# Routed two-expert layer: per-chunk adds on GpSimd, and the last tile's transposes moved between two matmul halves

## The reference, cut to what matters

```python
def _moe2_ref(x, w_gate, w_noise, noise, w1, w2):      # N = 2304 tokens, D = 512, E = 8, F = 1024
    ...
    for e in range(E):
        for k in range(2):
            mask = top2[:, k] == e
            h = np.maximum(x[mask] @ w1[e], 0.0)
            out[mask] += top2_w[mask, k, None] * (h @ w2[e])
```

## Time and profile before

| | us |
|---|---|
| three runs | 1079.15, 1078.52, 1079.46 |
| their median | 1079.15 |
| the profiled execution's own time | 1079.31 |
| its span, first to last instruction | 1077.5 |
| PE busy | 1064.3 (99%) |
| DVE, ACT, POOL busy | 584.1, 332.9, 386.0 |
| granted clock of PE, mean | 0.999 of full speed |

### The profile page before, as it was taken

The page is one execution under the profiler, slowest core; times in us unless marked ns, Lnnn a source line. Parts: engine busy times, 40 slices in busy tenths (PEclk is TensorE's granted clock), DMA queues, the critical chain, the costliest instruction groups (busy, mean ns, idle before and its releaser), DMA issues.

```text
span 1077.5 us, 20101 instructions
## 1 busy us (share of the span) xinstructions
PE 1064.3 (99%) x6053; PEld 932.2 (87%) x6054; DVE 584.1 (54%) x1212; ACT 332.9 (31%) x735; POOL 386.0 (36%) x358
## 2 busy tenths in 40 slices
PE   8989999999999999999999999999999999999997
PEld 7878999999999999999988888888888888888886
DVE  6777334364363463453457775555565555556553
ACT  7997223242342432432352111020303020110222
POOL 4557991030030030120185425070706142240486
PEclk9999999999999999999999999999999999999999
DMA  8876535411311311211084535172616344332576
GB/s 228 272 239 207 172 92 184 130 60 28 119 59 30 117 59 30 97 59 30 25 252 158 154 89 165 39 209 44 195 49 162 81 123 124 87 94 49 158 238 238
DMA packets 199635, 133.18 MB, mean 124 GB/s; under 512 B 128752, under 2 KB 161408, under 8 KB 199584
## 3 DMA queue, kind: packets, MB, share of 16 engines
q1 hardware_dynamic: 177728, 75.14, 25.7%
q10 hardware_dynamic: 16032, 38.47, 11.2%
q0 software_dynamic: 5824, 18.95, 5.1%
HBM read 85.87 MB, written 42.73 MB: 119 GB/s over the span
## 4 chain that ended last, share of the span: by engine, by line
PE 97%; ACT 1%; DVE 1%; issue 0%; DMA 0%; SPq 0%; ACTq 0%
PE bank L863 28%; PE bank L1023 22%; PE bank L1044 22%; PE bank L895 14%; PE bank L1057 3%; PE bank L807 2%; PE bank L834 2%; PE bank L817 1%; PE bank L801 1%; ACT p_sb L1197 1%; PE bank L940 1%; DMA k_sb<-in_kT 0%; PE bank L919 0%; PE bank L876 0%; DVE token_rows_b L1859 0%
## 5 line engine op out<-in xcount | busy, mean ns | idle before, releaser
L863 PE MATMUL bank<-x_parts,mlp_weights 128*128 128x384 f32 x1704 | 309.3, 336 | 0.0
L863 PEld LDWEIGHTS bank<-x_parts,mlp_weights 128*128 128x128 f32 x1704 | 298.2, 188 | 5.3
L1023 PE MATMUL bank<-expert_parts,xT_high 128*128 (+1 forms) x688 | 216.5, 396 | 0.0
L1044 PE MATMUL bank<-expert_parts,hT_high 128*128 (+1 forms) x688 | 212.1, 389 | 1.4 <-DVE hT_low L1785 1.4
L722 POOL TENSOR_TENSOR expert_parts<-raw_expert_a,expert_parts 128x512 fp32r<-128x512 f32 x64 | 81.5, 1306 | 234.6 <-ACT expert_parts L1362 232.3
L895 PE MATMUL bank<-mlp_weights,hidden_parts 128*128 128x512 f32 x648 | 162.0, 394 | 0.0
L1044 PEld LDWEIGHTS bank<-expert_parts,hT_high 128*128 128x128 f32 x688 | 129.0, 188 | 28.6 <-issue 2.0
L1023 PEld LDWEIGHTS bank<-expert_parts,xT_high 128*128 128x128 f32 x688 | 125.7, 188 | 24.4 <-issue 0.4
L895 PEld LDWEIGHTS bank<-mlp_weights,hidden_parts 128*128 128x128 f32 x648 | 120.1, 188 | 23.2 <-issue 1.0
L1023 PE MATMUL bank<-expert_parts,xT_low 128*128 (+1 forms) x344 | 134.3, 390 | 0.0
L1044 PE MATMUL bank<-expert_parts,hT_low 128*128 (+1 forms) x344 | 134.1, 390 | 0.0
(11 more groups left out here) (214 smaller groups left out, 1232.1 us busy)
## 6 DMA issues: line engine op xcount, KB each, us to landing
raw_expert_a<-in_w ACTq DMA_DIRECT2D x32, 512.0 KB
raw_expert_b<-in_w ACTq DMA_DIRECT2D x32, 512.0 KB, 4.2
x_row<-routed_rows SPq DMA_DIRECT2D x172, 64.0 KB
expert_rows<-y_row SPq DMA_DIRECT2D x43, 256.0 KB
expert_rows<-zeros SPq DMA_DIRECT2D x4, 2304.0 KB, 11.3
v_sb<-in_v SPq DMA_DIRECT2D x32, 256.0 KB, 3.5
q_sb<-in_qT SPq DMA_DIRECT2D x15, 288.0 KB, 3.7
k_sb<-in_kT SPq DMA_DIRECT2D x15, 288.0 KB, 4.0
```

The source lines that it names most:

```text
L863: last = nc.tensor.matmul(bank[:, 0:CHUNK], w_sb[:, i, wp, at:at + P], xp[:, par, part, k, :], start=n == 0, stop=n == 3 * KB - 1)
L1023: last = nc.tensor.matmul(ps[half][:, 0:512], (xTh, xTl)[xp][:, buf, k, :], ew_sb[:, bass.ds(slot, 1), wp, k * F2 + half * 512:k * F2 + ha ...
L1044: last = nc.tensor.matmul(y_bank(t)[:, 0:D], (hTh, hTl)[hp][:, f, :], ew_sb[:, bass.ds(slot, 1), 2 + wp, f * D:(f + 1) * D].rearrange("p a ...
```

## The change

The diff in full but for the semaphores' declarations (`second_in` now has six, `last_second_in` and `last_mixed` are gone, `second_tile_half_done` is called `half_done`):

```diff
@@ POOL
             for c in range(CHUNKS):
-                if c == CHUNKS - 1:
-                    add(c - 1)
                 stored = entry(pool, T_NEED + c, 16 * 64)
                 pool.wait_ge(places, 1)
                 pool.wait_ge(y_row_out, stored)
-                if c < CHUNKS - 1:
-                    gather_chunk(c, 1, second_in[c])
-                else:
-                    for t in range(CHUNK_TILES):
-                        gather(chunk_rows(c, 1)[:, t, :], slots_u[:, CHUNK_TILES * c + t, 1:2], last_second_in[t])
+                gather_chunk(c, 1, second_in[c])
                 if c + 2 < CHUNKS:
                     gather_chunk(c + 2, 0, first_in[c + 2])
-                if 1 <= c < CHUNKS - 1:
-                    add(c - 1)
+                if c < CHUNKS - 2:
+                    add(c)
+            add(CHUNKS - 2)
+            add(CHUNKS - 1)
@@ PE
-            return ps[4] if isinstance(t, int) and t == 2 else ps[5]
+            return ps[4] if isinstance(t, int) and t in (2, ETILES - 1) else ps[5]
...
-                if not (isinstance(t, int) and t in (0, 2)):
+                if not (isinstance(t, int) and t in (0, 2, ETILES - 1)):
                     pe.wait_ge(y_row_done, ONE + t)
...
-            tile(ETILES - 2, (ETILES - 2) % 2)
-            now = tile(ETILES - 1, (ETILES - 1) % 2)
-            pe_hT(pe, ETILES - 1)
-            pe_down2(pe, ETILES - 1, *now)
+            before = tile(ETILES - 2, (ETILES - 2) % 2)
+            t = ETILES - 1
+            now = entries(t)
+            pe_hT(pe, t - 1)
+            pe_up2(pe, t, t % 2, *now)
+            pe_down2(pe, t - 1, *before, (0,))
+            pe_hT(pe, t)
+            pe_down2(pe, t - 1, *before, (1,))
+            pe_down2(pe, t, *now)
@@ ACT
+            def store_chunk(c):
+                act.wait_ge(rows_added, CHUNK_TILES * (c + 1))
+                act.dma_start(out_rows(c), chunk_rows(c, 1)).then_inc(rows_out, 16)
+
             for c in range(CHUNKS):
-                if c < CHUNKS - 1:
-                    scale(c, 1, second_in, second_scaled)
+                scale(c, 1, second_in, second_scaled)
                 if c + 2 < CHUNKS:
                     scale(c + 2, 0, first_in, first_scaled)
-                if c >= 1:
-                    act.wait_ge(rows_added, CHUNK_TILES * c)
-                    act.dma_start(out_rows(c - 1), chunk_rows(c - 1, 1)).then_inc(rows_out, 16)
+                if c < CHUNKS - 2:
+                    store_chunk(c)
+            store_chunk(CHUNKS - 2)
             c = CHUNKS - 1
             for t in range(CHUNK_TILES):
-                act.wait_ge(last_mixed, t + 1)
+                act.wait_ge(rows_added, CHUNK_TILES * c + t + 1)
                 act.dma_start(out_rows(c)[:, t, :], chunk_rows(c, 1)[:, t, :]).then_inc(rows_out, 16)
@@ DVE
-                if isinstance(t, int) and t == 2 and b == 0:
-                    dve.wait_ge(second_tile_half_done, 1)
+                if isinstance(t, int) and t in (2, ETILES - 1) and b == 0:
+                    dve.wait_ge(half_done, 1 if t == 2 else 2)
...
             dve_hT(dve, t - 1)
             dve_relu(dve, t)
+            dve_hT(dve, t, (0,))
             dve_y(dve, t - 1)
-            dve_hT(dve, t)
+            dve_hT(dve, t, (1,))
             dve_y(dve, t)
-            dve.wait_ge(first_scaled, CHUNK_TILES * CHUNKS)
-            for t in range(CHUNK_TILES):
-                dve.wait_ge(last_second_in[t], 16)
-                n, row = CHUNK_TILES * c + t, chunk_rows(c, 1)[:, t, :]
-                nc.vector.scalar_tensor_tensor(out=row, in0=row, scalar=kept[:, 1, n:n + 1],
-                                               in1=chunk_rows(c, 0)[:, t, :], op0=ALU.mult, op1=ALU.add
-                                               ).then_inc(last_mixed, 1)
```

More of the change, by code:

```diff
@@ L346, in attention_moe_kernel @@
         tile_done = sem("tile_done")
-        second_tile_half_done = sem("second_tile_half_done")
+        half_done = sem("half_done")
         y_row_done = sem("y_row_done")
@@ L354, in attention_moe_kernel @@
         first_in = [sem(f"first_in_{i}") for i in range(CHUNKS)]
-        second_in = [sem(f"second_in_{i}") for i in range(CHUNKS - 1)]
-        last_second_in = [sem(f"last_second_in_{t}") for t in range(CHUNK_TILES)]
-        last_mixed = sem("last_mixed")
+        second_in = [sem(f"second_in_{i}") for i in range(CHUNKS)]
         first_scaled = sem("first_scaled")
@@ L1047, in pe_down2 @@
                         n += 1
-            last.then_inc(tile_done if halves[-1] == 1 else second_tile_half_done, 1)
+            last.then_inc(tile_done if halves[-1] == 1 else half_done, 1)
         def pe_hT(pe, t):
```

## The result

The changed kernel's median is 1080.7 us (22 runs, 1079.62 to 1083.26) against 1079.64 for the kernel before (22 runs, 1078.52 to 1080.87). The ratio is 1.0014, with a 95% interval of 1.0008 to 1.0019: 1.1 us slower at the first, small but clear of noise. The forecast was 1.4 us faster, with nearly all its chance on "the same" or better, and the time lies above its range. The profiled execution took 1082.46 us, with a span of 1080.6.

A forecast was written before the change was run, and what follows sets the result against it. It took PE (99% busy), then the tail through DVE's adds and the last store, with POOL's gathers close beside, as the bound. The earlier PE and POOL ends let stores finish 1.4 us sooner: 1079.15 - 1.4 = 1077.7 us, range 1076.2 to 1079.7.

The forecast's parts named there:

- the first part: Opening on what bounds the kernel: PE 99% busy, then DVE's adds, the last store at 1075.0, SP's wait until 1077.0.
- part 3: Stores at the end: output data finishes near 1075.15 instead of 1076.55, 1.4 us gained.
- Part 1: Tile 42's transposes move between the halves of tile 41's product; PE's last matmul ends at 1070.5, 1.7 us earlier.
- a shorter PE tail alone would run into their landing: At the end, PE finishing sooner would still meet the landing of chunk 5's second rows, gathered at 1067.57 to 1071.0.
- Part 2: POOL's adds follow their own chunk; chunk 5's adds end at 1073.36, last store issued at 1073.39, 1.6 us earlier.
- Nothing moves: POOL's adds of chunks 0 and 1: chunk 1's is ready at 1029.73, when POOL was adding at 1029.79 anyway.
- No slack: Chunk 5's add at 1069.60: all three rows wait for one semaphore, so a later landing counts in full.
- A rule against the change: Skill's port-sharing rule: DVE's copy of tile 42 would block POOL's chunk 5 adds, adding 0.7 us, giving 1078.4; left out.
- Rival A: Short landings of second rows: chunks 3 and 4 land in 3.6 to 3.8 us, 0.9 faster, 1076.8; chance 0.20.
- Rival B: Long landings before POOL's adds of chunks 3 and 4: 2.45 us more, 1080.2; chance 0.16.
- Rival C: Only the last landing or the output's backlog: chunk 4's store goes late, gain only 0.3 us, 1078.9; chance 0.08.
- D: Second bank's split comes late behind `dve_y(41)`, PE idles again; POOL still decides, 1077.7 stays; no chance given.

The follow-up runs named there:

- first session: The changed kernel's first 22 runs against the kernel before: 1080.7 us, ratio 1.0014.
- in the second: The changed kernel, nothing altered, run again for a second trace: 1083.17 us (5 runs), ratio 1.0038 to the kernel before.
- single executions: The changed kernel, nothing altered, three more times with one run and a trace each: 1083.12, 1083.56 and 1085.61 us.
- transposes alone: The kernel before with only the diff's PE part and its DVE part, the three scale-and-adds still on DVE: 1080.15 us, ratio 1.0005.

## Why the prediction was wrong

**The step that failed** is in the first part: "SP leaves its wait at 1077.0, 0.5 before the span's end". From it I took the last store as what sets the end, and in part 3 gained 1.4 us by making that store earlier. Two things ended there at once. SP's wait was one; POOL's drain, over at 1077.2, was the other, and the change moves exactly POOL's last instruction, from 1071.0 to 1073.4 by my own working. With the drain in the sum it reads 1073.4 + 6.1 + 0.2 = 1079.7 against 1077.5: 2.2 us slower instead of 1.4 faster. Measured were 1.1 us slower in the first session, 3.2 in the second and 2.5 to 5.0 in the single executions. So the drain turns the sign; the size then hangs on when the last add ends. Some 0.5 us of the distance to the forecast is none of the change's: the forecast started from a median of 1079.15 in three runs, and 22 runs gave 1079.64.

Point by point:
- Part 1 was right: PE's end and tile 42's copy came 1.6 us earlier (1.7 said). It was cover that made it worthless, and "a shorter PE tail alone would run into their landing" is what the kernel with the transposes alone shows.
- Part 2's chain came out within 0.6 us in the first trace and the second (969.2 and 969.9 against 969.6), and 2.2 to 4.8 us short in the three single executions. In the first trace that is in part luck: it started 1.7 us earlier, because tile 37 was copied earlier, and lost 0.9 of that on chunk 1. "Nothing moves" for chunk 1 was wrong in four of the five traces: its landing of 3.79 was one trace's. Of the other two that were taken over, chunk 3's (4.39) is in the middle of what the five traces gave and chunk 4's (4.20) at the low end. "No slack" was right as a warning, but the largest overruns were on chunks 2 and 3: 7.0 and 6.2 us in the slowest trace.
- Part 3: in the first trace the stores were through at 1076.7, or 1075.1 by the clock of before: the working gives about 1075.6 (data to 1075.15, and the wait left 0.4 behind them). The stores' gain was 1.9 us where 1.4 were said, and they were no longer the last.
- "A rule against the change", which I left out of the sum, would have put 0.7 us on the adds. Nothing of that shows: six adds took 7.49 us with tile 42's copy, out of PSUM, in the middle of them, which is twice 3.75.
- Rival A didn't happen: chunks 3 and 4 took 4.0 us and more in each of the five traces. Rival B did in the three single executions, on top of the drain: 2.2, 2.2 and 4.8 us, where its price was 2.45. The one trace of the first session doesn't show it. I gave it 0.16 and priced it on chunks 3 and 4 alone, while chunks 1 and 2 overran as well. Rival C couldn't show, as the stores no longer decide. D didn't happen.
- No rival held the real mechanism. The chain that ended last had PE and DVE at its end and no POOL, and the view by the block's own line would have shown the drain before the change was made.

## What to carry to other kernels

Ask of each engine when its queue is over, not only when its last useful work is: in this kernel POOL had to be done 6 us before the others, so its last work belonged on DVE, which has no such tail here, even where POOL is idle and DVE is not. Whether another kernel has this tail its own trace tells. Where two things end within 0.3 us of each other, price a change against both. And a wait for a transfer that the same queue has just issued is cheap by one trace's durations but carries the scatter of each landing into the end.

## What the runs showed of the hardware that I had not expected

- POOL's closing drain ends 6.0 to 6.2 us after POOL's last instruction in 13 of 14 traces, with adds, a memset of 0.12 us or a gather as the last. The other engines' drains after their last work are short: in the changed kernel ACT's takes 0.15 us, and DVE's is over 0.1 us after its last copy. What POOL does in that time, and whether a kernel without indirect transfers has it too, wasn't tried.
- Where a gather is the last, the drain may wait for it to land: in the kernel with the transposes alone the last row landed late (DVE's add at 1075.16) and the drain ended 7.1 us after the gather. One trace; it stays open.
- From the start of the third of three gathers of 256 KB to the scaling of their rows it takes 5.5 to 7.0 us for chunk 2 and 4.0 to 6.2 for chunk 3, in five traces of the same kernel.
- Tile 37's copy starts 2.2 to 2.3 us after the start of PE's last matmul of that tile in 13 of the 14 traces, and 0.5 us after it in the changed kernel's first trace. No run here settles why.
